# Two fused MoE layers on one Trainium2 core: eleven float32 output tiles instead of nine, ten last multiplications on GpSimd instead of four, and rewritten order tables

## What is computed

```python
# 1. causal convolution of 7 taps; taps are a softmax per head of 24 channels
w = softmax(weight)                                   # (8, 7)
x = einsum('hk,bskhg->bshg', w, windows_of_7(x))      # 8192 tokens x 192
# 2. first MoE layer
h = x @ w_in                                          # 192 -> 2048
x = (h * clip(h + 3, 0, 6) / 6) @ w_out               # 2048 -> 192
# 3. second MoE layer: a rational activation
h = x @ w_in2
P = a0 + a1*h + a2*h**2 + a3*h**3
Q = 1 + |b0|*|h| + |b1|*h**2
out = (P / (Q + 1e-6)) @ w_out2
```

## Time and profile before

| | |
|---|---|
| time, 3 executions | 1201.98 us median (1201.5 to 1202.02) |
| the profiled execution | 1204.0 us, its span 1201.9 us |
| TensorE busy | 1186.5 us, 99% of the span |
| VectorE | 1160.7 us, 97% |
| ScalarE, GpSimd | 1065.5 us (89%), 1072.9 us (89%) |
| DMA | 22.02 MB in all, 18 GB/s on average |

### The profile page before, as it was taken

How to read it: one execution, slowest core, us unless ns; L and a number is a source line. 1 busy time by engine, 2 the same in 40 slices (tenths; PEclk the granted TensorE clock), 3 DMA queues, 4 the chain that set the end, 5 groups by cost and what they waited for, 6 DMA issues and landing times. The chain is left out here.

```text
span 1201.9 us, 17842 instructions
## 1 busy us (share of the span) xinstructions
PE 1186.5 (99%) x5145; PEld 963.2 (80%) x5145; DVE 1160.7 (97%) x1784; ACT 1065.5 (89%) x1980; POOL 1072.9 (89%) x829
## 2 busy tenths in 40 slices
PE   8999999999999999999999999999999999999998
PEld 6778888888888888888888888888888888888754
DVE  7999999999999999999999999999999999998898
ACT  7888899898998988989998899889999899888886
POOL 5989989898998989999898998999989899898874
PEclk9999999999999999999999999999999999999999
DMA  4400000000000000010000000000000000000010
...
DMA packets 11313, 22.02 MB, mean 18 GB/s; under 512 B 1744, under 2 KB 3152, under 8 KB 11216
## 3 DMA queue, kind: packets, MB, share of 16 engines
...
...
## 5 line engine op out<-in xcount | busy, mean ns | idle before, releaser
L525 POOL TENSOR_TENSOR den<-den,sqr 128x512 f32<-128x512 f32 x246 | 360.7, 1466 | 92.3 <-ACT den L499 91.1
L599 POOL TENSOR_TENSOR g_lo<-g,g_hi 128x512 fp32r<-128x512 f32 x246 | 319.4, 1298 | 7.9 <-ACT g_hi L605 7.9
L492 POOL TENSOR_TENSOR g_lo<-r,g_hi 128x512 fp32r<-128x512 f32 x235 | 309.9, 1319 | 1.7 <-ACT g_hi L605 1.3
L605 ACT ACTIVATE g_hi<-g 128x512 fp32r<-128x512 f32 x246 | 155.9, 634 | 54.9 <-PE y1b_acc L385 47.1
L529 ACT ACTIVATE rsq<-den 128x512 f32<-128x512 f32 x246 | 155.0, 630 | 45.6 <-POOL den L525 42.7
L519 DVE SCALAR_TENSOR_TENSOR num<-h,monic,num 128x512 f32<-128x512 f32 x246 | 184.6, 751 | 8.2
L513 DVE SCALAR_TENSOR_TENSOR num<-h,monic,sqr 128x512 f32<-128x512 f32 x246 | 183.2, 745 | 0.0
L552 DVE SCALAR_TENSOR_TENSOR h<-num,monic,h 128x512 f32<-128x512 f32 x238 | 178.3, 749 | 0.2
L478 DVE SCALAR_TENSOR_TENSOR r<-r,h 128x512 f32<-128x512 f32 x235 | 160.4, 683 | 14.2 <-ACT r L471 13.4
L545 DVE SCALAR_TENSOR_TENSOR den<-den,h 128x512 f32<-128x512 f32 x238 | 161.9, 680 | 1.0 <-ACT h L541 0.9
L574 DVE SCALAR_TENSOR_TENSOR g<-den,h 128x512 f32<-128x512 f32 x238 | 161.1, 677 | 0.2
...
## 6 DMA issues: line engine op xcount, KB each, us to landing
...
```

The source lines that it names most:

```text
L492: eng.tensor_tensor(g1_lo[t % 2][:, :], gated(t)[:, :], f32(g1_hi[t % 2][:, :]), ALU.subtract).then_inc(S["g1lo"], 1)
L525: eng.tensor_tensor(den_of(t), den_of(t), sqr_of(t), ALU.add).then_inc(S["den_sum"], 1)
L599: eng.tensor_tensor(g2_lo[t % 2][:, :], g2[t % 2][:, :], f32(g2_hi[t % 2][:, :]), ALU.subtract).then_inc(S["g2lo"], 1)
L605: return eng.activation(dst, src, ACT.Copy)
```

## The change

- In the last block: `FULL` lists the tiles, counted back from tile 255, whose out product is float32. It had nine, now eleven. `LAST_STEP_GPSIMD` lists those whose `g_neg` is done by GpSimd; it had four, now ten.
- The first six full tiles take their weights from free columns of the three staging buffers, loaded one block earlier behind a semaphore of their own.
- The `monic_*` operations move from the START table to BEGIN (iterations 12 to 17 instead of 5 to 11); those with two tensor inputs become `tensor_scalar` with a column as constant, and two of them become one.
- The 24 warming matmuls are all 128 rows by 512 columns; before, the last six had 256 columns and three others 64 rows.
- The order tables of all stages change. RAMP ends at p = 28 instead of 30, and MIDDLE is used up to p = 258 instead of 257.
- `g_neg` waits in another order (the same semaphores).

```diff
 START "vector":
-    [("monic_side", 5), ("monic_safe", 6), ..., ("gate1", 0), ..., ("conv_b1", AHEAD, (2, 2, 2, 3, 5, 6, 7), 1), ("g1lo", 1),
-     ("conv_a", AHEAD, (0, 3, 5, 7, 8, 10))]
+    [("gate1", 0), ("conv_b1", AHEAD, (2, 2, 2, 3, 5, 6, 7), 1), ("g1lo", 1), ("conv_a", AHEAD, (2, 3, 5, 7, 8, 10))]
...
 RAMP "vector":
-    ... ("g1lo", 2), ("num1", 1), ("g_neg", 2), ("gate1", 0), ("newton", 1), ("g_first", 1)]
+    ... ("g1lo", 2), ("num1", 1), ("gate1", 0), ("g_neg", 2), ("newton", 1), ("g_first", 1)]
 MIDDLE "scalar":
-    [..., ("conv_a_first", AHEAD, -1), ("y1a_out", SUM1, 0), ("rsq2", 1), ("relu1", 0), ("x2a_hi", SUM1, 0), ...
+    [..., ("conv_a_first", AHEAD, -1), ("cs_a_hi", AHEAD, 10), ("rsq2", 1), ("y1a_out", SUM1, 0), ("x2a_hi", SUM1, 0), ("relu1", 0), ...
 MIDDLE "vector":
-    [("num2", 1), ("x2b_res", SUM1, 0), ("x2b_lo", SUM1, 0), ("num1", 1), ...
-     ("newton", 1), ("cs_b_lo", AHEAD, 10, 1), ("conv_a", AHEAD, (1, 4, 5, 6, 7, 8)), ...
+    [("num2", 1), ("x2b_res", SUM1, 0), ("num1", 1), ("x2b_lo", SUM1, 0), ...
+     ("newton", 1), ("conv_a", AHEAD + 1, (1, 4, 5, 6, 7, 8)), ("cs_b_lo", AHEAD, 10, 1), ...
 END "scalar":
-    [("y2a_out", SUM2, -1), ("sq2", 0), ("rsq2", 1), ("y1a_out", SUM1, -3), ("abs2", 0), ... ("rec2", 1), ("less_two", 2), ...
+    [("x2a_hi", SUM1, -3), ("y1a_out", SUM1, -3), ("sq2", 0), ("abs2", 0), ("y2a_out", SUM2, -1), ("rsq2", 1), ("less_two", 2), ..., ("rec2", 1), ...
-FULL = (2, 3, 5, 6, 8, 9, 11, 12, 14)
-LAST_STEP_GPSIMD = (3, 6, 9, 12)
+FULL = (2, 3, 5, 6, 7, 9, 10, 11, 12, 13, 14)
+LAST_STEP_GPSIMD = (2, 3, 5, 6, 7, 9, 10, 11, 12, 13)
...
-        spent = [r1[0], r1[1], y_a[0], raw_a[1], x2b_rest]
+        D = DA + DB
+        spent = [st[:, BLK:BLK + 2 * D] for st in stage_w] + [r1[0], r1[1], y_a[0], raw_a[1], x2b_rest]
...
+            if k == NB - 3:
+                load_w_full(eng, in_stage, d_w_stage, ("w_in_done", 2 * n_chunks), ("w_out_done", 2 * n_chunks))
...
         def monic_c2(eng):
             after_monic(eng, 3)
-            eng.tensor_tensor(c2, a2, a3_inverse, ALU.mult).then_inc(S["monic"], 1)
+            eng.tensor_scalar(c2, a2, a3_inverse, None, ALU.mult).then_inc(S["monic"], 1)
...
-            for i in range(WARM):
-                rows, cols = P if i < WARM - 9 or i >= WARM - 6 else DB, BLK if i < WARM - 6 else HALF
-                eng.matmul(h1_of(H_BANKS - 1)[0:rows, 0:cols], ones[:, 0:rows], ones[:, 0:cols],
-                           start=True, stop=True)
+            for _ in range(WARM):
+                eng.matmul(h1_of(H_BANKS - 1), ones[:, 0:P], ones[:, :], start=True, stop=True)
```

More of the change, by code:

```diff
@@ L562, in g_neg @@
                 return
[L563 to L564 removed]
+            if eng is nc.gpsimd:
+                eng.wait_ge(S["less_two"], gpsimds(t))
             if t - 2 in full:
```

111 lines of the change are left out of this document (56 added, 55 removed).

## The result

The changed kernel takes 1212.17 us (median of 4 runs, 1212.05 to 1212.54), the kernel before 1202.0 us in the same comparison (4 runs, 1201.5 to 1202.79). The ratio is 1.0085, with a 95% interval of 1.0067 to 1.0102: slower by some 10 us, where 4 us less were predicted.

The account below looks back on a forecast made before the run. TensorE was taken as the bound in the middle, with idle time only at both ends. Gains of 0.5 + 0.3 + 0.8 + 0 + 2.4 = 4.0 us gave 1198.0 us, range 1195.5 to 1200.8.

Parts of the forecast that it names:

- The middle: 14 block boundaries between the ramp and the tail: reordered copies and taps would cost 0, covered by margins of 0.4 us and more.
- The part on `y1a_out`, `rsq2` and `relu1`: Block boundaries: `y1a_out` ends 0.53 us later, leaving 0.42 us margin; `relu1` moves 0.5 us later but its `gate1` margin widens.
- Rival (d): Middle: moved taps meet GpSimd's reads, delaying `den_sum` and `y1a_out`; TensorE stops 14 times, 7 us lost, 1205.0 us; chance 0.07.
- Warming and the clock, 0.5: Start: longer warming matmuls leave less idle time, perhaps keeping TensorE's clock up; 0.5 us gained, bounds 0 and 1.1.
- Displaced tap and set-up, 0.3: First tiles: a tap moves behind the second `g1lo`, four `monic` operations leave VectorE's queue; 0.3 us gained, bounds 0 and 0.3.
- BEGIN's swap of `g1lo` and `x2b_lo`: Chain to the stop at 56 to 59 us: two operations swap places, the last keeps its time; counted 0.
- RAMP, 0.8: Ramp: `gate1` ahead of an older `g_neg` shortens two TensorE stops, by 0.59 and 0.2 us; 0.8 gained, bounds 0 and 1.7.
- before 75 us: Sign for the start: the forecast is wrong there if TensorE's in product of tile 24 starts no earlier than 75 us.
- The tail, 2.4: Last block: two more float32 tiles and six `g_neg` moved off VectorE; 2.4 us gained, bounds 3.1 gained and 1.6 lost.
- predicted 40.4: Sign for the tail: first float32 tile to last matmul takes about 40.4 us for 42.85, VectorE below 40 busy, GpSimd at 32.
- Rival (c): Tail: GpSimd becomes the bound, ten waits of 0.3 us for `g_neg` eat the gain; 1200.4 us; chance 0.15.

## Why the prediction was wrong, point by point

The ledger against the median of before, from the runs alone: start and BEGIN +1.0 (new forms -0.45, START's orders +0.7, BEGIN's +0.65, the set-up's place +0.1), ramp +0.4, middle +9.5, tail -0.85. Sum +10.0 us; measured +10.2. The middle is firm. The tail's part agrees with its trace (60.4 us for 61.2 from the in product of tile 239 to the last matmul). The parts of the start and the ramp are uncertain by 0.1 to 0.2 us each, since they are differences between medians of different comparisons.

- **The middle, "Cost: 0, covered by margins of 0.4 us and more": the step that failed.** Its sentence on the taps was "Taps arrive at two other iterations, whose margins are wider than that." It set the tap's 0.66 us against a margin of TensorE, and taken alone that comparison holds for the stop that cost most: the margin is 0.96 us. But it is not all that the tap does. VectorE has no gap there to work the 0.66 us off, so they are still missing at tile 48, where 0.60 us was the margin (3.1 us in all), and the tap changes when later instructions meet GpSimd's. One such meeting stood at 0.07 us in the trace of before, and I didn't list which VectorE instructions start within a tenth of a us of a GpSimd one. Lost, it adds 1.1 us to the 0.67, more than the margin (6.4 us in all). Measured: 9.5 us for 0. The part on `y1a_out`, `rsq2` and `relu1` held: no wait for `y_a` in the middle, in any run.
- **`x2b_lo` behind `num1`** was among the edits that I gave nothing in the middle. Alone it costs 2.5 us; in the changed kernel the late tap hides it.
- **Rival (d)** had the mechanism, a VectorE and a GpSimd instruction that exclude each other, and nearly the price (7 us for 9.5), but the wrong meeting and the wrong victim. It let the tap meet `x2a_lo` and made `y1a_out` late; the waits it named never came. A tap at the boundary does hold the `den_sum` behind it, as the rival said and against its own argument: in the changed kernel that tap starts at 345.50, `den_sum` at 345.60 and takes 1.80 us. But `y1a_out` of that boundary started at 342.30 and was long done. Its time, 1205.0, is 7 us short: 4.0 of gains that aren't there, 0.5 lost at the ends, and 2.5 of price.
- **Warming and the clock, 0.5**: 0. The granted clock did stay at 1.0, as the step hoped, and the trace of before suggested up to 1.1 us; but the median of before has no such episode, so nothing was to be gained against it. The sum was made against the profiled execution and then moved by the 2.0 us between it and the median; those 2.0 us were this very episode, so 0.5 us of it was counted twice. The hypothesis that less idle time keeps the clock up fits the traces: in the three with the low clock the warming matmuls take 6.45 to 6.64 us and TensorE is idle for 1.10 to 1.28 us behind them, in the 16 others they take 7.31 us or more and at most 0.36 us is idle. That the longer matmuls would end 0.7 us later and delay nothing was wrong by more: they end at 10.77 for 9.05, and the first real matmul starts at 10.61 for 10.15. Little came of that, since TensorE's next stop, at 11.9 us, was shorter by nearly as much (0.21 us, for 0.61 in the kernel before with the new middle).

```profile
2.43 8.34 PE L1071 MATMUL h<-x1a_hi 128*128 128x512 f32 x24 [2.43 <-POOL x1a_hi L1132]
```

- **Displaced tap and set-up, 0.3**: the set-up's new forms give 0.45, the tap takes 0.7. "I count 0" for BEGIN's swap of `g1lo` and `x2b_lo` was 0.65 lost with `w_out_hi` ahead of `conv_b_first`, of which the prediction said nothing.
- **RAMP, 0.8**: about 0.4 lost. The step took for granted that what `gate1` is handed over in VectorE's queue reaches TensorE. The stop before tile 24 is still there:

```profile
74.69 0.50 PE L370 MATMUL h<-x0a_hi,win_hi 128*128 128x512 f32 x1 [0.85 <-DVE r L484]
```

  It starts before 75 us, as the prediction asked, yet against a start at full clock (73.88) it is late. A bound in absolute time was no test.
- **The tail, 2.4**: 0.85. From the first float32 tile to the last matmul the window is 41.22 us for 42.85, predicted 40.4. VectorE is below 40 us busy, as said, and GpSimd at 31.35 for 32:

```profile
1165.24:1206.46 41.22, 41.22 (x125) 20.00 (x123) 38.33 (x59) 33.67 (x64) 31.35 (x25) 1.00 0.00 1
```

  TensorE now has no idle time there, so its own work was undersized: a tile with its in product takes 3.22 us from start to start (1168.45 to 1171.67), not 1.96 + 1.14 = 3.10, since each change between the two forms starts slowly (0.33 us between the first two starts, 1167.19 and 1167.52). It was so before the change too, where the in product behind a float32 tile takes 1.26 us (1167.79 to 1169.05), so of the 4.75 us that the prediction held for idle some 1.1 were work. The other 0.7 us were lost ahead of that window. The wait for `y2a_out` grew by 1.1 us there; the prediction saw it move ("now stands behind `sq2` and `abs2` (1 us)") and charged nothing. Put back, it gives 0.3 us; where the rest is lost was not tried. Rival (c) did not come: TensorE waits for no `g_neg` of GpSimd.
